# Chunks of 384 tokens, attention in two PSUM banks, means of the second batch on the vector engine, and products of zeros at the start, in an attention and two-network kernel

## What is computed

```python
k_sum = k.reshape(B, H, nb, block, D).max(axis=3)
v_sum = v.reshape(B, H, nb, block, D).mean(axis=3)
scores_all = concat([where(mask_l, scale * q @ k.T, -1e9), scale * q @ k_sum.T + log(block)])
a = softmax(scores_all)
attn = a @ concat([v, v_sum])
h = maximum(attn @ w_in, 0.0)          # 1536 tokens x 512 -> 2048
x = h * h @ w_out                      # -> 512
h = x @ w_in2                          # -> 1024
solu = h * softmax(h)
out = (solu - mean) / sqrt(var + 1e-6) * g_ln @ w_out2
```

## Time and profile before

| | |
|---|---|
| median of three runs | 515.67 us |
| profiled execution, its time | 513.74 us |
| its span | 512.0 us |
| TensorE busy | 490.3 us, 96% |
| vector engine busy | 250.7 us, 49% |
| ACT busy | 219.5 us, 43% |
| GpSimd busy | 45.6 us, 9% |
| DMA | 39.38 MB, mean 77 GB/s |

### The profile page before, as it was taken

One profiled execution on the slowest core, in us unless ns is written; L12 is line 12 of the kernel. 1 busy time (PEld: TensorE's weight loads), 2 busy tenths in 40 slices (PEclk: granted clock), 3 DMA queues, 4 the chain that ended last, 5 costly groups with the idle time before them and its releaser, 6 DMA issues.

```text
span 512.0 us, 9826 instructions
## 1 busy us (share of the span) xinstructions
PE 490.3 (96%) x3936; PEld 451.0 (88%) x3936; DVE 250.7 (49%) x504; ACT 219.5 (43%) x573; POOL 45.6 (9%) x65
## 2 busy tenths in 40 slices
PE   2678999999999999999999999999999999999997
PEld 2458999999999999999999999999988888888885
DVE  3438878744445434544345433456764444444340
ACT  2357677444343343544445432344443333333331
POOL 1123445100000200000000000000000000000000
PEclk9989999999999999999999999999999999999999
DMA  8484763231102100030002002223221221000011
GB/s 274 164 252 126 203 214 114 72 135 57 58 27 89 38 24 25 17 109 27 27 27 84 1 1 83 84 83 96 77 76 61 70 84 34 20 22 20 22 41 41
DMA packets 26397, 39.38 MB, mean 77 GB/s; under 512 B 1824, under 2 KB 13216, under 8 KB 26352
## 3 DMA queue, kind: packets, MB, share of 16 engines
q1 hardware_dynamic: 26352, 38.76, 23.4%
HBM read 31.41 MB, written 7.34 MB: 76 GB/s over the span
## 4 chain that ended last, share of the span: by engine, by line
PE 91%; DVE 5%; issue 1%; ACT 1%; DMA 1%; POOL 0%; DVEq 0%; ACTq 0%
PE bank L760 26%; PE bank L735 26%; PE bank L855 12%; PE bank L828 12%; PE bank L681 5%; PE bank L694 3%; PE bank L724 3%; PE bank L709 3%; PE bank L843 2%; DVE probs L526 1%; DVE neg_max L530 1%; DMA k_raw<-kT 1%; ACT probs L384 1%; DVE probs L541 1%; DVE solu L643 1%
## 5 line engine op out<-in xcount | busy, mean ns | idle before, releaser
L735 PE MATMUL bank<-x_hi,win_hi 128*128 128x256 f32 x384 | 110.6, 288 | 0.7 <-POOL win_lo L347 0.7
L760 PE MATMUL bank<-h_hi,wout_hi 128*128 128x256 f32 x384 | 109.2, 284 | 0.2
L760 PE MATMUL bank<-h_lo,wout_hi 128*128 128x256 f32 x384 | 108.6, 283 | 0.0
L760 PE MATMUL bank<-h_hi,wout_lo 128*128 128x256 f32 x384 | 108.6, 283 | 0.0
L735 PE MATMUL bank<-x_hi,win_lo 128*128 128x256 f32 x384 | 108.5, 283 | 0.0
L735 PE MATMUL bank<-x_lo,win_hi 128*128 128x256 f32 x384 | 108.5, 283 | 0.0
L553 DVE TENSOR_TENSOR sqr<-relu 128x256 f32<-128x256 f32 x96 | 44.5, 464 | 102.0 <-ACT relu L426 102.0
L426 ACT ACTIVATE relu<-bank 128x256 f32<-128x256 f32 x96 | 36.6, 381 | 103.6 <-PE bank L735 102.4
L735 PEld LDWEIGHTS bank<-x_hi,win_hi 128*128 128x128 f32 x384 | 73.5, 191 | 1.6 <-POOL win_lo L347 1.2
L760 PEld LDWEIGHTS bank<-h_hi,wout_hi 128*128 128x128 f32 x384 | 73.6, 192 | 1.4 <-issue 1.3
L760 PEld LDWEIGHTS bank<-h_lo,wout_hi 128*128 128x128 f32 x384 | 73.7, 192 | 0.0
(11 more groups left out here) (69 smaller groups left out, 700.4 us busy)
## 6 DMA issues: line engine op xcount, KB each, us to landing
v_ext<-vwin SPq DMA_DIRECT2D x24, 188.0 KB
win_raw<-w_in_t SPq DMA_DIRECT2D x8, 512.0 KB, 13.8
wout_raw<-w_out_t SPq DMA_DIRECT2D x8, 512.0 KB, 13.0
win_raw<-w_t SPq DMA_DIRECT2D x8, 512.0 KB, 3.5
k_raw<-kT SPq DMA_DIRECT2D x8, 399.0 KB, 6.3
q_sb<-qT SPq DMA_DIRECT2D x24, 128.0 KB, 3.8
out<-o_sb SPq DMA_DIRECT2D x12, 256.0 KB, 2.0
y_dram<-x_hi SPq DMA_DIRECT2D x4, 512.0 KB, 3.1
```

Of the source, the lines that this page charges most:

```text
L735: last = nc.tensor.matmul(up_bank(n), win[a][:, f * WC + k * P:f * WC + (k + 1) * P], x[b][:, c % 2, k * CH:(k + 1) * CH], start=(k == 0 a ...
L760: last = nc.tensor.matmul(down_bank(d), wout[a][:, f * WC + d * P:f * WC + (d + 1) * P], h[b][:, n % 3, :], start=(f == 0 and a == 0 and b ...
```

## The change

Chunks have 384 tokens, so the first network has 4 chunks and 64 steps, with products of 384 columns. A unit has 3 tiles, so 192 queries; there are 32 units, 8 to a chunk. The outputs of `down` take banks 2 to 5, one each; in the loop attention has banks 0 and 1 (the third transpose goes beside the scores), and in the start it has more. PE does values, transposes, scores in a slot; ACT's `copy_last` takes the third transposed tile once the next unit's scores are read. 8 units stand ahead of the loop. `load_vw` now has 94 rows of 1536 bytes.

The means of the second batch are sums by DVE (`sums_v`, four quarters of the dimensions, then `mean_v`) of a load with 96 rows of 4096 bytes (`vblk`), and SP spreads the result with four DMAs (`spread_v`). `keep_busy` makes products of zeros on PE ahead of `scores(0)`, of `scores(1)` and of `means(0)`. `chunk_y` and `save_y` go by quarters, and `sqr` shares the memory of `h_lo`.

```diff
--- before.py
+++ after.py
-CH = 256
...
+CH = 384
...
+TPU = 3
+UQ = TPU * QT
+RB = S // UQ
+HPC = CH // UQ
+UNITS = B * RB * PPB
+UPB = RB * PPB
+UPC = HPC * PPB
 UC = TPU * KX
 STEPS = NCHUNK * F1
 LAST = (NCHUNK - 1) * F1
...
-SLOTS = {0: (None, 4, 5), 4: (4, 5, 6), 7: (5, 6, 7), 10: (6, 7, 8), 13: (7, 8, 9)}
-for _u in range(8, UNITS):
-    SLOTS[4 * (_u - 4)] = (_u, _u + 1 if _u + 1 < UNITS else None, _u + 2 if _u + 2 < UNITS else None)
+SLOTS = {0: (None, 8, 9), 2: (8, 9, 10), 4: (9, 10, 11), 5: (10, 11, 12), 7: (11, 12, 13), 9: (12, 13, 14),
+         10: (13, 14, 15), 12: (14, 15, 16), 13: (15, 16, 17)}
+for _u in range(2 * UPC, UNITS):
+    SLOTS[2 * (_u - UPC)] = (_u, _u + 1 if _u + 1 < UNITS else None, _u + 2 if _u + 2 < UNITS else None)
...
+X_AT = {x_step(u): u for u in range(UPC, UNITS)}
+
+V_AT = {6: 0, 8: 1, 10: 2, 12: 3}
...
-        sb(early, "wout_first", [P, (F1 - PPB * SK * P // WC) * WC], F32)
+        idle = sb(early, "idle", [P, (F1 - PPB * SK * P // WC) * WC], F32)
...
-            def load_vn(p):
-                sp.dma_start(v_next[:, p % 2, :], vrows[PPB + p, :, :]).then_inc(vn_in[p % 2], 16)
+            def load_vn(j):
+                if j:
+                    sp.wait_ge(vsum_ok, j)
+                sp.dma_start(v_next[:, :], vblk[j, :, :]).then_inc(vn_in, 16)
+
+            def spread_v(p):
+                src = v_mean[p * NB:(p + 1) * NB, :].unsqueeze(1).to_broadcast([NB, TPU, P])
+                sp.dma_start(v_ext[0:NB, p, :].rearrange("p (t d) -> p t d", t=TPU), src).then_inc(vs_in[p], 16)
...
-            sp.dma_start(mask[:, :], mask_c).then_inc(mask_in, 16)
+            sp.dma_start(mask[:, 0:UC], mask_c[:, 0:UC]).then_inc(mask_in, 16)
             load_k(0, 1)
             load_q(1)
             sp.dma_start(ident[:, :], ident_c).then_inc(ident_in, 16)
             load_k(0, 2)
             load_q(2)
             load_vf(0)
+            load_vw(0)
             load_k(0, 3)
             load_q(3)
-            load_vw(0)
             load_vf(1)
             load_vw(1)
-            load_w(win_raw, w_in_t, 0, win_in)
+            sp.wait_ge(scores_ok, 1)
+            load_q(4)
             load_vf(2)
             load_vw(2)
+            sp.wait_ge(scores_ok, 2)
+            load_q(5)
+            load_w(win_raw, w_in_t, 0, win_in)
             load_vf(3)
             load_vw(3)
+            sp.dma_start(mask[:, UC:], mask_c[:, UC:]).then_inc(edge_in, 16)
+            sp.wait_ge(scores_ok, 3)
+            load_q(6)
+            sp.wait_ge(scores_ok, 4)
+            load_q(7)
+            for p in range(PPB):
+                sp.wait_ge(attn_ps, p + 1)
+                load_vw(PPB + p)
             load_w(wout_raw, w_out_t, 0, wout_in)
             load_w(win_raw, w_in_t, 1, win_in)
-            sp.wait_ge(scores_ok, 1)
-            load_q(4)
-            sp.wait_ge(scores_ok, 2)
-            load_q(5)
+            sp.dma_start(g_sb[:, :], g_cols).then_inc(g_in, 16)
+            sp.wait_ge(scores_ok, 5)
+            load_q(8)
+            sp.wait_ge(scores_ok, 6)
+            load_q(9)
             load_w(wout_raw, w_out_t, 1, wout_in)
             load_w(win_raw, w_in_t, 2, win_in)
-            sp.dma_start(g_sb[:, :], g_cols).then_inc(g_in, 16)
-            sp.wait_ge(scores_ok, 3)
-            load_q(6)
-            load_w(win_raw, w_in_t, 3, win_in)
-            load_w(wout_raw, w_out_t, 2, wout_in)
-            sp.wait_ge(attn_ps, 1)
-            load_vw(4)
-            sp.wait_ge(attn_ps, 2)
-            load_vw(5)
-            load_w(win_raw, w_in_t, 4, win_in)
-            load_w(wout_raw, w_out_t, 3, wout_in)
-            sp.wait_ge(scores_ok, 4)
-            load_q(7)
-            sp.wait_ge(attn_ps, 3)
-            load_vw(6)
-            sp.wait_ge(attn_ps, 4)
-            load_vw(7)
-            for g in range(5, F1 // WG):
+            for p in range(PPB):
+                if p >= 2:
+                    sp.wait_ge(scores_ok, PPB + p + 1)
+                    load_q(UPC + p)
+                sp.wait_ge(attn_ps, PPB + p + 1)
+                load_vw(UPC + p)
+            for g in range(3, F1 // WG):
                 load_w(win_raw, w_in_t, g, win_in)
                 load_w(wout_raw, w_out_t, g - 1, wout_in)
+                if g == 5:
+                    load_vn(0)
             load_w(wout_raw, w_out_t, F1 // WG - 1, wout_in)
-            load_vn(0)
-            load_vn(1)
...
+            for u in range(UPC, UNITS):
+                if u >= 2 * UPC and u % UPC == 0:
+                    save_y(u // UPC - 2)
                 sp.wait_ge(attn_ps, u + 1)
                 if u + PPB < UNITS:
                     load_q(u + PPB)
                     load_vw(u + PPB)
...
+                if UPC + 2 < u < UPC + 2 + VP:
+                    load_vn(u - UPC - 2)
+                if u == UPB - 1:
+                    sp.wait_ge(vavg_ok, 1)
+                    for p in range(PPB):
+                        spread_v(p)
 
...
+            nc.gpsimd.memset(idle[:, 0:2 * P], 0.0).then_inc(idle_ok, 1)
             nc.gpsimd.memset(minus_half[:, :], -0.5).then_inc(half_ok, 1)
             for p in range(PPB):
                 windows_k(p)
                 summaries_k(0, p)
-            windows_k(4)
+            for u in range(PPB, UPC):
+                windows_k(u)
             w_in_low(0)
             w_in_low(1)
-            windows_k(5)
+            windows_k(UPC)
             w_in_low(2)
             w_in_low(3)
+            windows_k(UPC + 1)
             for n in range(LAST):
                 if n + 4 < F1:
                     w_in_low(n + 4)
...
-                nc.scalar.copy(probsT[0:KX, u % 2, :], probsT_bank).then_inc(probsT_ok, 1)
+                if u < UPC:
+                    nc.scalar.copy(probsT[0:KX, u % 2, :], bank[0:KX, 1 + 2 * (u % 2), 0:TPU * P])\
+                      .then_inc(probsT_ok, 1)
+                else:
+                    nc.scalar.copy(probsT[0:KX, u % 2, 0:2 * P], bank[0:KX, 1, 0:2 * P])
+
+            def copy_last(u):
+                act.wait_ge(masked_ok, min(u + 2, UNITS))
+                nc.scalar.copy(probsT[0:KX, u % 2, 2 * P:3 * P], turned_bank(u, 2)).then_inc(probsT_ok, 1)
...
+                if u >= UPC:
+                    act.wait_ge(probsT_ps, min(u + 2, UNITS))
+                if u >= 2 * UPC:
+                    act.wait_ge(y_saved[u % PPB], 32 * (u // UPC - 1))
...
             exps(0)
             exps(1)
+            copy_mean(0)
             copy_probsT(0)
+            copy_probsT(1)
+            x_high(0)
             exps(2)
-            copy_probsT(1)
-            copy_mean(0, 0)
             exps(3)
-            x_high(0)
+            copy_mean(1)
+            copy_mean(2)
+            x_high(1)
             copy_probsT(2)
-            copy_mean(0, 1)
             w_in_high(0)
-            x_high(1)
-            copy_mean(0, 2)
             w_in_high(1)
             x_high(2)
+            exps(4)
+            copy_mean(3)
+            exps(5)
             copy_probsT(3)
-            copy_mean(0, 3)
+            copy_probsT(4)
+            x_high(3)
+            copy_probsT(5)
+            x_high(4)
             w_out_high(0)
-            x_high(3)
-            exps(4)
+            exps(6)
+            x_high(5)
+            exps(7)
+            copy_probsT(6)
+            x_high(6)
+            copy_probsT(7)
+            x_high(7)
             w_in_high(2)
+            exps(8)
             hidden(0)
             w_in_high(3)
...
+                if n in SLOTS and SLOTS[n][1] is not None:
+                    copy_last(SLOTS[n][1])
                 if n + 2 < STEPS:
                     hidden(n + 2)
+                if n in SLOTS and SLOTS[n][2] is not None:
+                    exps(SLOTS[n][2])
...
+            def sums_v(j):
+                dve.wait_ge(vn_in, 16 * (j + 1))
+                nc.vector.tensor_reduce(v_sum[:, j * VD:(j + 1) * VD],
+                                        v_next[:, :].rearrange("p (d b) -> p d b", b=BLOCK), AX.X, ALU.add)\
+                  .then_inc(vsum_ok, 1)
+
+            def mean_v():
+                dve.wait_ge(vsum_ok, VP)
+                nc.vector.tensor_scalar_mul(v_mean[:, :], v_sum[:, :], 1.0 / BLOCK).then_inc(vavg_ok, 1)
...
                     chunk_y(n // F1 - 1)
+                if n in SLOTS and SLOTS[n][2] is not None:
+                    maxima(SLOTS[n][2])
                 if n in X_AT:
                     x_low(X_AT[n])
-                if n in SLOTS and SLOTS[n][2] is not None:
-                    maxima(SLOTS[n][2])
                 if n + 2 < STEPS:
                     hidden(n + 2)
-                if n - 1 in SLOTS and SLOTS[n - 1][2] is not None:
-                    normalise(SLOTS[n - 1][2])
-                if n - 2 in SLOTS and SLOTS[n - 2][2] is not None and UPB <= SLOTS[n - 2][2] + 1 < UPB + PPB:
-                    sums_k(1, SLOTS[n - 2][2] + 1 - UPB)
+                if n in SLOTS and SLOTS[n][2] is not None:
```

(62 more changed lines are left out.)

252 lines of the change are left out of this document (138 added, 114 removed).

## The result

The changed kernel took 527.89 us (median of 4 runs, 526.5 to 528.41), the kernel before beside it 514.75 (4 runs, 513.1 to 515.68): ratio 1.0255, 95% interval 1.0217 to 1.0292. It is slower by 13 us, and 1.9 us above the top of the predicted range. The profiled execution took 526.5 us with a span of 524.7, where 516.8 had been worked out for it: 9.7 more.

A forecast was written before the change was run, and what follows sets the result against it. Bound by chains and loads at the start, then by TensorE's instruction stream. 61.8 + 258.5 + 38.0 + 6.5 + 0.6 = 365.4 us to h2(0), +3.1 in all against before: forecast 518.7 us, range 502 to 526.

The forecast's parts named there:

- part 2: Attention slots in the loop, units of three tiles: 1.65 us a slot, 23 slots, 38.0 us.
- part 3: Second batch's means moved to VectorE: 6.4 us less on TensorE, their loads and spreads costed at nothing.
- Products of 384 columns: First network's matmuls: 0.1737 us each, 266.8 us for 276.5, so 9.7 us less.
- Rival E: First network's matmuls: a product goes by columns alone, 0.180 us, nothing saved; 528.4 us, chance 0.02.
- Rival D: Start: vwin loads cost by rows, wout group 0 lands at 55.2; 528.1 us, chance 0.05.
- Start: Before the loop: narrow vwin loads delay wout group 0 to 45.8 us; steady loop begins at 61.8, for 44.1 before.
- rival B: Start: same mechanism, landing at 44.0 and a warmer chain behind; within 0.5%, 514.9 us, chance 0.25.
- rival A: Start: vwin loads don't hold back wout group 0, loop begins between 43 and 51; 499.9 to 507.9 us, chance 0.2.
- stalls of the loop: TensorE's waits at slots 5, 10, 13 and VectorE's load, 6.5 us, plus 0.6 for x_low at chunk boundaries.
- Zeros at nothing: Products of zeros at the start: costed at nothing, between -2 and +1.5 us.
- Behind h2(0): After the second network's start: products of the two steps left grow by 1.3 us, its own work unchanged.
- Rival C: Loop, steps 9 to 13: VectorE becomes the bound, 5 to 8 us more; 525.2 us in the middle, chance 0.15.

The follow-up runs named there:

- v96: The changed kernel with vwin and its load widened from 94 to 96 rows (two rows of zeros nothing reads): 515.57 us, ratio to before 1.0029.
- act_late: The changed kernel with w_out_high(0) behind x_high(7) on ACT and w_out_low(0) moved accordingly on VectorE: 523.18 us, ratio 1.0187.
- early94: The changed kernel, vwin loads still 94 rows, with SP issuing wout group 0 and win group 1 ahead of vwin loads 4 to 7: 522.73 us, ratio 1.0181.
- slot_order: The changed kernel with the loop's slots turned back to values, scores, transposes: 525.57 us, ratio 1.021.
- all4: The changed kernel with v96, v_next loads ahead of k loads on SP, pool_first and slot_order together: 501.29 us, ratio 0.9757.
- all4_nz: all4 without the products of zeros: 501.18 us.
- no_zeros: The changed kernel without the three keep_busy calls and their wait: 525.9 us, ratio 1.0235.
- pool_first: The changed kernel with windows_k ahead of w_in_low in GpSimd's loop list: 519.39 us, ratio 1.0108.
- all5: all4 plus early94's order on SP and, on GpSimd, windows_k(9) ahead of w_in_low(2) and (3): 491.35 us, ratio 0.9559.

## Why the prediction was wrong

Two steps failed: the price of a slot in part 2 (1.65 us summed, 1.93 measured, 6.4 us over 23 slots), and the v_next loads in part 3, put at nothing, where the second of them was the first wait of slot 10 (7.0 us lost there, 2.6 summed). By its own sum, h2(0) was forecast for 365.4 and came at 374.92:

- **Products of 384 columns: right.** 0.1733 us against 0.1737; 62 steps 0.4 us less than summed. Rival E falls; that its time (528.4), like that of D (528.1), lies close to the measured one is chance.
- **Start: right in mechanism, 1.6 us too long.** wout group 0 landed at 44.05 for 45.8, scores(9) ended at 60.19 for 61.8 (16.1 us behind the landing, 16.0 summed), and v96, act_late and early94 show that the narrow loads do it. The landing is that of rival B (44.0), whose warmer chain did not come. VectorE's 8.69 us for the mask are not in the walk; that leaving them out did no harm to the number is partly luck. Rival D's landing of 55.2 falls. So does rival A's premise, that the loads don't hold wout group 0 back; with wide loads the loop began at 49.7, within A's 43 to 51.
- **Slots: the largest miss, 6.4 us** (23 times 0.28). Part 2 took "three quarters of the first three and all of the rest" from rows in which the transposes stand behind the scores, though the change puts them ahead. 0.18 of the 0.28 is that order, shown by slot_order; 0.10 is that a group of three quarters takes more than three quarters (values 0.50 for 0.465, scores 0.75 for 0.72, and the ends). The 0.38 for four transposes stands in no row shown; the next product begins 0.41 behind them, which changes the sum by under 0.01 a slot.
- **The v_next loads: costed at nothing, the second miss.** "Its followers are needed over 15 us later" was said of the first load. The second waits behind a k load on SP, which waits for windows_k(14), which waits behind w_in_low. Of the stalls of the loop, 7.1 us had been summed (6.5 and 0.6); what the trace leaves is 374.92 - 60.19 - 258.1 - 44.4 = 12.2: slot 5 2.25 (forecast 2.6, as GpSimd's queue says), slot 10 7.0 (forecast 2.6), slot 13 0.6 (forecast 0.9), 2.0 in the first step, and 0.2 in its first product behind scores(9).
- **The clock at the head of the loop: left out, these 2.0 us.** The prediction priced one scores group cold, but not the first up and down behind it.
- **Zeros at nothing: right**, by all4 and all4_nz (0.1 us apart); the pair of the changed kernel and no_zeros, 2.0 us apart with overlapping intervals, can't tell it so closely.
- **Behind h2(0): right.** The last two downs take 4.18 us as one piece, and the part from h2(0) on 149.8 us for 148.4, 1.4 more (1.3 forecast).
- **Rival C** does not hold: VectorE does release TensorE at slots 5, 10 and 13, but 4.86 us of its own time at slot 10 were a wait for a DMA, and in pool_first, with the same work, TensorE's wait there is 0.66.

Sum: -1.6 - 0.4 + 6.4 + 5.1 = 9.5, the difference at h2(0); 5.1 is 12.2 less the 7.1 that were summed. The range ended at 526 because the slot price had no bounds at all and slot 10 was priced from one queue alone.

The kernel all5 sums as the prediction would have it: 40.6 + 62 x 4.163 + 23 x 1.75 = 339.0, and h2(0) begins at 340.42. From scores(9) on it takes 299.8 us to h2(0), where the kernel before took 319.5 from its turned(4) at 44.1. Of these 19.7 us the steps are 12.6 (62 x 4.163 for 94 x 2.88) and the means that left TensorE 6.4. That the larger chunks pay is thus worked out from prices and not shown by a run, and in part the work only stands outside this stretch: more attention lies ahead of the loop, and the first and last steps are larger. That the kernel before could gain at its own start by the same kind of reordering was not tried; with 96 rows alone it gains nothing.

## What to carry to other kernels

A cost that is hidden is hidden by a margin: 1.6 us at the weights before, about 12 us that wider loads gave back, after four more of the same loads were put ahead. When work is moved or multiplied in one queue, write down for each waiting instruction what it waits for, what stands behind it, and follow that to the next queue (GpSimd to SP to VectorE here), also for the second and third of a row of loads. And price a group of matmuls by a row in which its neighbours are the same as in the new order.
